# The first pair of heads in an attention and feed-forward kernel: another order on three engines, one bank evicted by another engine, ten zero products for fourteen

## The reference

```python
q_rot, k_rot = rotate(q), rotate(k)                     # batch 4, heads 8, 576 tokens, 64 features
scores = q_rot @ k_rot.T / sqrt(64)
attn = exp(scores - max(scores)); attn = attn / (sum(attn) + 1e-9)
x = (attn @ v) as 2304 tokens x 512 features
x = (sigmoid(x @ w_gate) * (x @ w_val)) @ w_out         # 512 -> 1536 -> 512
h = x @ w_in                                            # 512 -> 1024
solu = h * softmax(h)
y = ((solu - mean) / sqrt(var + 1e-6) * g_ln) @ w_out2  # 1024 -> 512
```

## Time and profile before

| | |
|---|---|
| Median of 3 runs | 959.44 us (957.44 to 960.39) |
| Profiled execution, whole time | 958.99 us |
| Its span, first to last instruction | 957.2 us |
| TensorE matmul, busy | 943.4 us, 99% |
| VectorE, ScalarE, GpSimd, busy | 475.0, 371.3, 338.8 us |
| Mean granted TensorE clock | 0.997 of 2.4 GHz |
| Chain that ended last | TensorE 90%, DMA 3%, waiting for nothing shown 2% |

### The profile page before, as it was taken

How to read it: one execution, slowest core, us unless ns; L and a number is a source line. 1 busy time by engine, 2 the same in 40 slices (tenths; PEclk the granted TensorE clock), 3 DMA queues, 4 the chain that set the end, 5 groups by cost and what they waited for, 6 DMA issues and landing times.

```text
span 957.2 us, 15347 instructions
## 1 busy us (share of the span) xinstructions
PE 943.4 (99%) x5346; PEld 787.2 (82%) x5346; DVE 475.0 (50%) x859; ACT 371.3 (39%) x801; POOL 338.8 (35%) x246
## 2 busy tenths in 40 slices
PE   8999999999989999999999999999999999999998
PEld 6787888888777889888888888888888888888886
DVE  6787888788753243323324233243434554444441
ACT  6887888888853111111111111111111343333332
POOL 5455647465405805104203302401756432222200
PEclk9999999999999999999999999999999999999999
DMA  3435343343422100200100100100120011000112
GB/s 95 128 86 136 90 128 101 104 121 85 116 93 81 40 27 1 67 0 1 66 1 1 67 1 0 44 0 0 45 86 1 1 23 22 22 22 22 22 22 45
DMA packets 35810, 48.14 MB, mean 50 GB/s; under 512 B 6592, under 2 KB 22208, under 8 KB 35776
## 3 DMA queue, kind: packets, MB, share of 16 engines
q1 hardware_dynamic: 35632, 47.53, 18.1%
q10 hardware_dynamic: 144, 0.15, 0.1%
HBM read 33.02 MB, written 5.31 MB: 40 GB/s over the span
## 4 chain that ended last, share of the span: by engine, by line
PE 90%; DMA 3%; issue 2%; DVE 1%; ACT 1%; POOL 1%; SPq 1%; DVEq 0%; ACTq 0%; POOLq 0%
PE ps L1145 31%; PE ps L1189 15%; PE ps L1252 10%; PE ps L1227 9%; PE ps L1127 8%; PE ps L1085 7%; PE ps L1109 6%; PE ps L1237 2%; DMA rrep<-inverses 1%; PE ps L1053 1%; DMA inverses<-rinv_t 1%; PE ps L1024 1%; DMA raw_q<-in_q 1%; DVE nmax L889 0%; SPq L506 0%
## 5 line engine op out<-in xcount | busy, mean ns | idle before, releaser
L1145 PE MATMUL ps<-x_hi,w_hi 128*128 128x512 f32 (+1 forms) x480 | 177.0, 369 | 0.0
L1145 PE MATMUL ps<-x_lo,w_hi 128*128 128x512 f32 (+1 forms) x480 | 176.7, 368 | 0.0
L1145 PE MATMUL ps<-x_hi,w_lo 128*128 128x512 f32 (+1 forms) x480 | 176.6, 368 | 0.0
L953 DVE TENSOR_TENSOR hid<-ps,sig 128x512 f32<-128x512 f32 (+1 forms) x60 | 38.3, 638 | 243.1 <-PE ps L1145 214.6
L767 ACT ACTIVATE sig<-ps 128x512 f32<-128x512 f32 (+1 forms) x60 | 33.3, 555 | 299.6 <-PE ps L1145 299.6
L889 DVE TENSOR_REDUCE nmax<-ps 128x1 f32<-128x576 f32 x144 | 107.1, 752 | 37.7 <-PE ps L1085 37.6
L1085 PE MATMUL ps<-kT,qT 128*128 128x288 f32 x640 | 120.7, 314 | 3.0 <-ACT prob L735 2.2
L637 POOL TENSOR_SCALAR w_hi<-raw_w 128x1024 fp32r<-128x1024 f32 x15 | 41.3, 2775 | 215.5 <-PE ps L1189 215.5
L1085 PEld LDWEIGHTS ps<-kT,qT 128*128 128x128 f32 x640 | 89.5, 189 | 17.8 <-ACT prob L735 10.3
L1145 PEld LDWEIGHTS ps<-x_hi,w_hi 128*128 128x128 f32 x480 | 90.5, 189 | 15.4 <-issue 0.5
L1145 PEld LDWEIGHTS ps<-x_hi,w_lo 128*128 128x128 f32 x480 | 90.5, 189 | 15.0
(11 more groups left out here) (117 smaller groups left out, 1611.2 us busy)
## 6 DMA issues: line engine op xcount, KB each, us to landing
kT<-kT SPq DMA_DIRECT2D x30, 304.0 KB, 4.6
raw_k<-in_k SPq DMA_DIRECT2D x16, 288.0 KB, 3.8
raw_q<-in_q SPq DMA_DIRECT2D x16, 288.0 KB, 4.9
rrep<-inverses SPq DMA_DIRECT2D x16, 288.0 KB, 3.8
out_y<-y_sb SPq DMA_DIRECT2D x36, 128.0 KB, 2.3
v_sb<-in_v SPq DMA_DIRECT2D x64, 64.0 KB, 2.3
raw_w<-in_moe_w_gate SPq DMA_DIRECT2D x6, 512.0 KB, 3.7
raw_w<-in_moe_w_val SPq DMA_DIRECT2D x6, 512.0 KB, 4.6
```

The lines of the kernel that those rows point to most:

```text
L1145: last = nc.tensor.matmul(in_parts(gv_ps[f][n][:, 0:size(c)], c), w, x, start=m == 0, stop=m == len(todo) - 1)
```

## The change

Three lists of step 0 and the tuple `FILL` are written anew. The steps from 1 on, GpSimd's and SyncE's queues, and all that is computed stay as they were.

- On TensorE k is turned before S2 and no longer before S3; T behind S4 and no longer before it; A0 and B0 together behind S5; q behind S6; B2 behind S7 and A1 behind S8.
- ScalarE takes k's high part before exponential 2, evicts B2 and A1 behind exponential 7, both before exponential 8, and leaves A0 out.
- VectorE copies A0 (to `pT`, L897) between maxima 6 and 7, and takes the low part of T behind maximum 5 and that of q behind maximum 7.
- `turn_over(2)` stands behind k, S3, B0, q and S7: ten zero products for fourteen.

```diff
--- before.py
+++ after.py
@@ -250,9 +250,9 @@
         ORDER_POOL = ["RK", "RQ", "XL"]
 
         ORDER_SP = ["RW", "RR", "LK", "T", "LQ", "LV"]
-        FIRST_PE = ["S0", "S1", "S2", "k", "S3", "T", "S4", "B0", "S5", "q", "A0", "S6", "B2", "S7", "A1", "S8"]
-        FIRST_ACT = ["S0", "S1", "S2", "k", "S3", "T", "S4", "B0", "S5", "q", "A0", "S6", "B2", "S7", "A1", "S8"]
-        FIRST_DVE = ["S0", "S1", "S2", "S3", "k", "S4", "T", "S5", "S6", "q", "S7", "S8"]
+        FIRST_PE = ["S0", "S1", "k", "S2", "S3", "S4", "T", "S5", "A0", "B0", "S6", "q", "S7", "B2", "S8", "A1"]
+        FIRST_ACT = ["S0", "S1", "k", "S2", "S3", "T", "S4", "B0", "S5", "q", "S6", "S7", "B2", "A1", "S8"]
+        FIRST_DVE = ["S0", "S1", "S2", "S3", "k", "S4", "S5", "T", "S6", "A0", "S7", "q", "S8"]
         AHEAD = {"A2": -1, "A3": -1, "B1": -1, "B3": -1, "K": -1, "TQ": -1, "KT": -1, "RT": -1, "PV0": -1, "PV1": -1,
                  "INV": -1, "XL": -1, "k": 1, "q": 1, "T": 1, "RQ": 2, "RK": 2, "RW": -1, "RR": -1, "LK": 2, "LQ": 2,
                  "LV": 1}
@@ -1145,7 +1145,7 @@
                         last = nc.tensor.matmul(in_parts(gv_ps[f][n][:, 0:size(c)], c), w, x, start=m == 0, stop=m == len(todo) - 1)
                     last.then_inc(val_full if n else gate_full, 1)
 
-            FILL = ("S1", "S2", "S3", "S4", "S5", "S6", "S7")
+            FILL = ("k", "S3", "B0", "q", "S7")
             BETWEEN = {"KT": (0,), "TQ": (1, 2), "PV1": (3,)}
 
             def item(name, p, step):
```

## The result

| | before | changed |
|---|---|---|
| Median, 20 runs each | 957.73 us | 955.83 us |
| Lowest | 956.00 us | 954.09 us |
| Profiled execution, span | 957.2 us | 955.2 us |
| Ratio changed to before | | 0.9982, interval 0.9974 to 0.9991 |

The account below looks back on a forecast made before the run. TensorE, 99% busy, bounded the kernel; step 0 could gain by TensorE's path (1.9 us) or T's low part (1.26 less 0.66), the later deciding: 0.60 off, 958.4 or 958.84 by base, said 958.8; range 956.7 to 960.4.

Parts of the forecast that it names:

- the two chains: Step 0: the score-tile round (two tiles in 2.49 us), and SyncE's kT copies and raw_q load behind T's low part.
- k sooner, scores 3 to 5, the low part of T: Step 0: earlier rounds give 1.26 us, one more maximum costs 0.66, so SyncE's chain starts 0.60 earlier.
- TensorE's own path: Through step 0: TensorE stands before step 1's S0 at 27.2 us, 1.9 before its old 29.11.
- A0, four zero products, A1, GpSimd: Step 0: A0 and A1 nothing, zero products at most 0.9 us inside the 1.9, GpSimd covered by 5.69 us idle.
- What is late next: Step 1: TensorE waits 1.1 us at S0; landings keep their times, so T's turn is 0.60 earlier, 33.73 against 34.33.
- rival A: TensorE's own path decides if raw_q lands 1.7 us sooner; 1.2 to 2.3 gained, 957.1 to 958.2; chance 0.16.
- Rivals B and C: B: nothing gained, 959.4 us, chance 0.17; C: clock falls in step 0 and stays down, 963.9 us, chance 0.04.
- Rival D: One clock fall more, or the one at 280 us gone: 1.7 us either way, 957.1 or 960.5; chance 0.11.

Follow-up runs that it names:

- before_t_low_later: The kernel before with only T's low part moved behind maximum 5 on VectorE; 959.11 us, ratio 1.0013 (1.0002 to 1.0024).
- the late weights: First feed-forward weights loaded behind the inverse sums in step 15, rounded behind maximum 8: changed kernel 955.26 us (0.9969), kernel before 956.75 us (0.9987).
- k sooner: The kernel before with only k turned before S2 on TensorE and evicted before exponential 2 on ScalarE; 957.55 us, ratio 0.9995.

## Why the prediction was wrong, point by point

*What bounds the kernel, and the two chains:* right in the main. Moving the low part of T by a maximum either way moved the turn of T by -0.60 and by +2.0 (forecast 1.8), and taking raw_q out from behind it removed the wait in both orders. Two things were overlooked. The low part of T also frees the bank that the turn of q needs, so the two bounds are not independent: the later low part moved both. And the copy of kT did not gate S0 of step 1 in the kernel before.

*k sooner, scores 3 to 5, the low part of T:* right to 0.1 us at every place. The issue of the copies moved by 0.57 from S0 (+8.94 or +8.95 in every trace of before, +8.37 or +8.38 of the changed kernel), where 0.60 was forecast.

*TensorE's own path:* right. 1.9 forecast, 1.78 with the gate of raw_q out of both and some 0.2 still lost to the copy at S0.

*A0, four zero products, A1, GpSimd:* right that they give little. A0 nothing at the turn; the zero products 0.3 at the copies' issue, which the prediction had put inside the 1.9 and not on the chain. No clock was lost to them: it was granted in full in step 0 with ten zero products and with fourteen. The rule that the prediction took from the Trainium skill ("TensorE: Matmul & The Clock Gate", Part 1), that activity releases the clock, is not refuted by that. The clock did fall in step 0 of before_t_low_later (0.57 in 24 to 26 us), behind a wait of 1.42 us, which agrees with it; in the changed kernel no wait in step 0 was above 0.7.

*What is late next:* this step failed, the term of the landings, which was kept and moved. "The same transfers are issued in the same order, so I keep their times": the chain from issue to landing took 6.9 us on average in the five traces with the old lists (with and without the late weights), and 5.8 in the four with the new ones. At the turn of T that makes 1.66 us (mean +20.49 and +18.83): 0.57 by the issue, which was forecast, and 1.1 by the landings, which was not. The second copy's landing was kept too, at 5.3 us where it took 4.5, so that the forecast wait of 1.1 at S0 of step 1 was some 0.2. At the end of attention it is 2.0 (the turn of the inverse sums of step 15, +253.7 and +251.7 in the same traces), so nothing was given back. The forecast of 0.60 is this term short, and the measured 1.9 agrees with the whole. The bounds beside it did reach a gain of 2.3, as rival A: raw_q landing sooner. I gave it 0.16 because I took the landing for chance, and chance for as likely to be worse. The time fell into its bounds, but not by its mechanism: TensorE still waited for raw_q at T. The chain was 6.7 or 7.1 in every trace of the kernel before and 5.7 (once 6.2) in those of the changed one, which a single trace can't show.

*The base:* the sum was made against the median of three runs that lay 1.7 us above that of twenty. The range took in the spread of the time saved, but not the spread of the base, which the three runs had shown to be 2.95 us wide. With the later median as its base the same forecast reads 957.1.

*Rivals B and C:* did not come. *Rival D* is always there: the fall of the clock differs from run to run in both kernels. It does not make the gain: in runs with a mean granted clock of 0.999 or 1.000 the mean time is 956.74 us for before (28 runs) and 954.78 for the changed kernel (13), in those below it 958.62 (60) and 956.99 (18), 2.0 and 1.6 us apart at like clock (three chips for before, so this is a rough comparison).

## What to carry to other kernels

When a change shortens the work ahead of a DMA that others wait for, the DMA's time is a term of its own with a spread of its own; take it from several executions, and ask what else the same DMA engines carry at its new place. Better, take the load out from behind the step that gates it: that edit alone took the changed kernel from 956.21 us to 954.58 in the median (six runs of it; 0.8 to 1.3 sooner at the turn of T) and took the wait at T away, while on the kernel before it gave nothing that could be told, since there TensorE's own path was nearly as late. And a difference of 2 us in a kernel whose runs spread over 4 needs its base from many runs, or a place in the trace that can be compared, like the turn of T here.

## What the runs showed of the hardware

One transfer of 16 KB of instructions keeps a DMA engine for 0.9 to 1.4 us. In the traces in which it started with or inside the copies or the load, the chain was 6.7 to 7.4 us, against 5.6 to 5.9 with it outside (and 6.2 once), and its place repeats from run to run to 0.05 us, in one of two places for the kernel before (+10.0 and +13.3) and one for the changed (+9.1). That it is the cause of the longer chain is supported by the packets that began only as the transfer ended (k sooner and three traces of the old order), by one kernel whose copies landed in 5.3 or 4.4 us according to its place, and by fifteen traces of fifteen; no kernel of the study moved it alone. What the fetch hangs on stays open, and so does why a transfer that starts 0.4 us ahead of the packets and overlaps them does no harm.

The granted clock fell to its lower level, 1.2 GHz, in step 0 of one variant, with a mean of 0.57 in 24 to 26 us, after a wait of 1.42 us on TensorE. Between runs of one kernel such a fall, at the end of attention, was worth 1.9 us.

The issue of two copies took 1.14 us in most traces and 2.47 in one, which delayed the load behind them by 1.3 us; the load then landed in 3.7 us in place of 4.5.
